# Attention in two-head matmuls, with v fetched once and copied on the chip

## The reference

```
for c in range(24):
    k_full = concat(mem_k, k[c*32-16 : c*32+40])      # 8 + 56 = 64 keys (fewer at both ends)
    v_full = concat(mem_v, v[same window])
    scores = q_c @ k_full.T / 8
    a = softmax(scores)
    out[chunk c] = a @ v_full
```

## Time and profile before

| | us |
|---|---|
| median of three runs | 758.82 |
| the profiled execution, whole | 762.52 |
| its span | 760.8 |
| attention, to the end of the last L616 | 241.5 |
| first mixture, to the last L761 | 329.2 |
| TensorE busy over the span | 642.0 (84%) |
| VectorE, ScalarE, GpSimd busy | 332.4, 228.0, 184.6 |

### The profile page before, as it was taken

How to read it: one execution, slowest core, us unless ns; L and a number is a source line. 1 busy time by engine, 2 the same in 40 slices (tenths; PEclk the granted TensorE clock), 3 DMA queues, 4 the chain that set the end, 5 groups by cost and what they waited for, 6 DMA issues and landing times.

```text
span 760.8 us, 18972 instructions
## 1 busy us (share of the span) xinstructions
PE 642.0 (84%) x6916; PEld 357.9 (47%) x6917; DVE 332.4 (44%) x543; ACT 228.0 (30%) x616; POOL 184.6 (24%) x159
## 2 busy tenths in 40 slices
PE   5999999699998969766430899999989999999992
PEld 3566666366665526433100445445444545444441
DVE  2333334133434652156370465665555566531120
ACT  2422424042422220010020344443434443443341
POOL 2211101010102000004786032332332233322221
PEclk9998999599999989897655799999999999999997
DMA  7769677558539999999805836455454543343332
GB/s 154 221 163 187 173 193 182 160 139 194 93 60 308 106 317 395 397 408 409 313 10 124 175 42 152 58 137 120 79 139 62 120 78 52 44 52 41 43 48 33
DMA packets 120601, 117.51 MB, mean 154 GB/s; under 512 B 57600, under 2 KB 87088, under 8 KB 120544
## 3 DMA queue, kind: packets, MB, share of 16 engines
q1 hardware_dynamic: 109104, 93.80, 42.1%
q0 software_dynamic: 11440, 22.87, 19.8%
HBM read 91.79 MB, written 22.76 MB: 151 GB/s over the span
## 4 chain that ended last, share of the span: by engine, by line
PE 57%; DMA 21%; issue 10%; DVE 3%; SPq 3%; ACT 3%; POOL 0%; ACTq 0%; DVEq 0%; POOLq 0%
PE ps L831 21%; DMA out_dram<-logits,arena 9%; DMA out_dram<-comb,arena 9%; PE ps L553 9%; PE ps L587 7%; PE ps L616 7%; DMA arena<-in_moe_w_dram 3%; PE ps L572 3%; PE ps L822 2%; PE ps L655 2%; PE ps L732 1%; SPq L418 1%; SPq L433 1%; ACT arena L920 1%; PE ps L761 1%
## 5 line engine op out<-in xcount | busy, mean ns | idle before, releaser
L831 PE MATMUL ps<-arena 128*128 x1320 | 300.2, 381 | 4.3 <-issue 3.5
L831 PEld LDWEIGHTS ps<-arena 128*128 128x128 f16 x1320 | 125.8, 98 | 143.6 <-issue 11.4
L1385 DVE SCALAR_TENSOR_TENSOR arena<-ps,arena 128x1024 f16<-128x1024 f32 x55 | 67.3, 1224 | 171.4 <-ACT arena L998 171.4
L998 ACT ACTIVATE arena<-ps 128x512 f16<-128x512 f32 x110 | 59.7, 594 | 130.3 <-PE ps L822 130.3
L553 PE MATMUL ps<-ident 128*128 128x128 f16 x384 | 90.9, 237 | 0.6 <-issue 0.5
L587 PE MATMUL ps<-arena 64*32 64x64 f32 x1536 | 72.1, 248 | 11.1 <-issue 11.1
L531 POOL DMA_INDIRECT out_dram<-logits,arena x28 | 47.9, 1710 | 123.6 <-DMA out_dram<-comb,arena 75.1
L531 POOL DMA_INDIRECT out_dram<-comb,arena x27 | 47.8, 1770 | 115.5 <-DMA out_dram<-logits,arena 90.7
L616 PE MATMUL ps<-arena 64*32 64x64 f32 x1536 | 65.5, 228 | 5.2 <-ACT arena L920 5.0
L468 POOL COPY arena<-arena 128x768 f32<-128x768 f32 x32 | 26.5, 828 | 173.8 <-PE ps L572 156.1
L522 POOL DMA_INDIRECT slot_table<-arena,zeros x48 | 51.5, 1072 | 29.8 <-DVE zeros L1283 15.5
(11 more groups left out here) (212 smaller groups left out, 577.9 us busy)
## 6 DMA issues: line engine op xcount, KB each, us to landing
arena<-in_moe_w_dram SPq DMA_DIRECT2D x26, 2048.0 KB, 18.7
arena<-in_moe_w_dram SPq DMA_DIRECT2D x12, 1024.0 KB, 5.8
arena<-in_v_dram SPq DMA_DIRECT2D x32, 308.0 KB
out_dram<-zeros POOLq DMA_DIRECT2D x2, 3200.0 KB, 18.7
arena<-in_q_dram SPq DMA_DIRECT2D x16, 384.0 KB, 4.5
arena<-in_k_dram SPq DMA_DIRECT2D x16, 384.0 KB, 5.0
arena<-arena SPq DMA_DIRECT2D x16, 128.0 KB
slot_table<-trow POOLq DMA_DIRECT2D x1, 935.0 KB, 38.1
```

Source lines behind the costliest of these rows:

```text
L831: last = mm(psY[par], hT[par][:, ph, c, :], W2[:, bass.ds(expert, 1), pw, c, :].rearrange("p o n -> p (o n)"), start=(c == 0 and ph == 0 a ...
L998: nc.scalar.activation(hT[par][:, 0, 4 * n:4 * n + 4, :].rearrange("p c n -> p (c n)"), psH[par][:, n, :], ACT.Relu).then_inc(relu_act, 1)
L1385: V.scalar_tensor_tensor(out=hT[i % 2][:, 1].rearrange("p c n -> p (c n)"), in0=psH[i % 2].rearrange("p a n -> p (a n)"), scalar=0.0, in1= ...
```

## The change

The two heads of a pair go into one matmul. `kB` holds the keys of head 0 in its rows 0 to 63 and of head 1 in rows 64 to 127, in two separate column ranges with zeros in the other half; `qT` has both heads in its 128 rows. A score matmul is now 128 rows by 32 columns with 2 x 56 columns moving. Six further matmuls with 128 columns of `qT` as the stationary operand give the scores of the 2 x 8 memory keys (`mkB`). `vB` is laid out in the same block-diagonal way, so that the product with v is 24 matmuls with 128 columns moving. The windows in `kB` need no copies of overlapping keys. The `keep_clock` matmuls are gone.

v is fetched in blocks of 64 tokens, each row once, 1536 packets per pair, which serves the even or odd chunks directly; the blocks of the other chunks are copied from it by VectorE (head 0) and ScalarE (head 1), new function `move_v`. The memory values are spread by GpSimd in two dependent copies (`spread_memv` moves there from VectorE). `qT`, `kB` and `aT` are single buffers. `load_v` now waits for the product of the pair two before; its first call waits until `vB` is zeroed.

```
-                sp.wait_ge(memv_spread, g + 1)
+                if not (isinstance(b, int) and b == 0 and m < 2):
+                    sp.wait_ge(pv_done, g - 1)
...
-                            (vW[i][lo + NM:lo + KEYS, 1:CH - 1, :],
-                             bass.AP(v_h.tensor, base + (CHUNK - LEFT) * D,
-                                     [[D, WIN], [CHUNK * D, CH - 2], [1, D]])),
+                            (vB[i][lo:lo + 64, EV + 1:VB - 1, own],
+                             bass.AP(v_h.tensor, base + (64 - NM - LEFT) * D,
+                                     [[D, 64], [64 * D, EV - 1], [1, D]])),
...
+            def spread_memv(b, m, after):                    # GpSimd
+                g, i = b * PPB + m, m % 2
...
+                pool.wait_ge(v_moved_dve, g + 1)
+                pool.wait_ge(v_moved_act, g + 1)
+                pool.wait_ge(memv_loaded[i], (b * (PPB // 2) + m // 2 + 1) * 32)
+                pool.wait_ge(k_ordered, after)
...
+                nc.gpsimd.tensor_copy(vB[i][0:NM, 0:CH, 0:D],
+                                      mvn[i][0:NM, :].unsqueeze(1).to_broadcast([NM, CH, D])
+                                      ).then_inc(memv_half, 1)
+                pool.wait_ge(memv_half, g + 1)
...
+                nc.gpsimd.tensor_copy(vB[i][64:64 + NM, 0:CH, D:2 * D],
+                                      mvn[i][64:64 + NM, :].unsqueeze(1).to_broadcast([NM, CH, D])
+                                      ).then_inc(memv_spread, 1)
...
             with pool.Fori(1, B) as b:
                 for m in range(PPB):
                     reorder(b, m)
+                    spread_memv(*((b, m - 2) if m >= 2 else (b - 1, m + PPB - 2)), b * PPB + m + 1)
+            spread_memv(B - 1, PPB - 2, PAIRS)
+            spread_memv(B - 1, PPB - 1, PAIRS)
             pool.wait_ge(scores_done, PAIRS)
...
-                    for h in range(2):
-                        lo = h * 64
-                        last = mm(psS[j * Q:(j + 1) * Q, h, t, :], qT[i][lo:lo + 64, c * CHUNK:(c + 1) * CHUNK],
-                                  kW[i][lo:lo + 64, c + 1, :], start=True, stop=True)
-                    if c % 2 == 0:
-                        keep_clock(2)
+                for t in range(ST):
+                    mm(psS[:, t // 3, t % 3, :, 0:NM], qT[:, t * P:(t + 1) * P],
+                       mkB[:, :, bass.ds(g * NM, NM)], start=True, stop=True)
...
+                    last = mm(psS[j * Q:(j + 1) * Q, t // 3, t % 3, :, NM:KEYS],
+                              qT[:, c * CHUNK:(c + 1) * CHUNK], kB[:, :, c * CHUNK:c * CHUNK + WIN],
+                              start=True, stop=True)
...
+                pe.wait_ge(memv_spread, g + 1)
...
+                    last = mm(psO[j * Q:(j + 1) * Q, t // 3, t % 3, :, :], aT[:, c * CHUNK:(c + 1) * CHUNK],
+                              vB[i][:, c // 2 + (1 - c % 2) * EV, :], start=True, stop=True)
...
+            def move_v(b, m):                                # ScalarE; VectorE does the same for head 0
+                i = m % 2
+                act.wait_ge(v_loaded[i], (b * (PPB // 2) + m // 2 + 1) * 96)
+                nc.scalar.copy(vB[i][64:96, 0:EV, D:2 * D], vB[i][96:128, EV:VB - 1, D:2 * D])
+                nc.scalar.copy(vB[i][96:128, 0:EV, D:2 * D], vB[i][64:96, EV + 1:VB, D:2 * D]
+                               ).then_inc(v_moved_act, 1)
...
+            V.memset(at(11, 0, 2 * PADDED), 0.0)
+            V.memset(mkB, 0.0).then_inc(kw_zeroed, 1)
+            V.memset(at(3, 0, 2 * VB * P), 0.0).then_inc(vb_zeroed, 1)
```

More of the change, by code:

```diff
@@ L342, in load_memv @@
                 i = m % 2
-                if isinstance(b, int) and b == 0 and m < 2:
-                    sp.wait_ge(mvn_zeroed, 2)
-                else:
+                if not (isinstance(b, int) and b == 0 and m < 2):
                     sp.wait_ge(memv_spread, g - 1)
@@ L464, in reorder @@
                     pool.wait_ge(done, (g + 1) * 16)
+                    if n == 0 and not first:
+                        if not (isinstance(b, int) and b == 0 and m < 3):
+                            pool.wait_ge(memv_spread, g - 2)
                     if not first:
@@ L613, in attend @@
                     t, j = c // CPT, c % CPT
-                    for h in range(2):
-                        lo = h * 64
-                        last = mm(psO[j * Q:(j + 1) * Q, h, t, :],
-                                  aT[lo:lo + 64, c * CHUNK:(c + 1) * CHUNK],
-                                  vW[i][lo:lo + 64, c, :], start=True, stop=True)
-                    if c % 2 == 0:
-                        keep_clock(6)
+                    last = mm(psO[j * Q:(j + 1) * Q, t // 3, t % 3, :, :], aT[:, c * CHUNK:(c + 1) * CHUNK],
+                              vB[i][:, c // 2 + (1 - c % 2) * EV, :], start=True, stop=True)
                 last.then_inc(pv_done, 1)
@@ L874, in _ @@
         def _(act):
+            act.wait_ge(kw_zeroed, 1)
             act.wait_ge(mkT_done, 1)
-            nc.scalar.copy(mkT[:, :], ps[:, 2, 0:P]).then_inc(mkT_ready, 1)
-            act.wait_ge(mkT_ready, 1)
+            for h in range(2):
+                own = slice(h * 64, h * 64 + 64)
+                nc.scalar.copy(mkB[own, h, :], ps[own, 2, 0:P]).then_inc(mkT_ready, 1)
             def copy_q(b, m):
                 g, i = b * PPB + m, m % 2
-                if not (isinstance(b, int) and b == 0 and m < 2):
-                    act.wait_ge(scores_done, g - 1)
+                if not (isinstance(b, int) and b == 0 and m < 1):
+                    act.wait_ge(scores_done, g)
                 for x in range(2):
@@ L931, in step @@
                     copy_k(*after)
-            act.wait_ge(kw_zeroed, 1)
+                if not (last and m == PPB - 1):
+                    move_v(*((b, m + 1) if m + 1 < PPB else (b + 1, 0)))
             copy_q(0, 0)
@@ L938, in _ @@
             exp(0, 0)
+            move_v(0, 0)
             for m in range(PPB):
@@ L1091, in step @@
                 norm(b, m)
-                if not (last and m >= PPB - 2):
-                    spread_memv(*((b, m + 2) if m + 2 < PPB else (b + 1, m + 2 - PPB)))
-            def spread_memv(b, m):
-                g, i = b * PPB + m, m % 2
-                dve.wait_ge(memv_loaded[i], (b * (PPB // 2) + m // 2 + 1) * 32)
-                V.tensor_copy(vW[i], mvn[i].unsqueeze(1).to_broadcast([P, CH, D])).then_inc(memv_spread, 1)
-            for i in range(2):
-                V.memset(mvn[i], 0.0).then_inc(mvn_zeroed, 1)
-            V.memset(at(11, 0, 2 * (CH + 2) * KEYS), 0.0).then_inc(kw_zeroed, 1)
-            dve.wait_ge(mvn_zeroed, 2)
-            spread_memv(0, 0)
-            spread_memv(0, 1)
+                if not (last and m == PPB - 1):
+                    move_v(*((b, m + 1) if m + 1 < PPB else (b + 1, 0)))
+            V.memset(at(11, 0, 2 * PADDED), 0.0)
+            V.memset(mkB, 0.0).then_inc(kw_zeroed, 1)
+            V.memset(at(3, 0, 2 * VB * P), 0.0).then_inc(vb_zeroed, 1)
+            move_v(0, 0)
             softmax(0, 0)
```

99 lines of the change are left out of this document (59 added, 40 removed).

## The result

The changed kernel takes **693.2 us** (median of 4 runs, 691.2 to 694.7) against 758.0 of the kernel before, measured with it: ratio 0.913, 95% interval 0.907 to 0.920. The forecast was 689, the range 666 to 722. The profiled execution took 692.8, with a span of 691.0. A few microseconds can only be compared within one series. Medians are over all executions of a kernel; the ratios leave out those that took over 1.5% more than its fastest.

A forecast was written before the change was run, and what follows sets the result against it. Attention was taken as bound by TensorE alone, DMA next. Old span 760.8, less 83.1 saved in attention, plus 11 given back, is 688.7, with 1.7 around it 690; median forecast 689 us, range 666 to 722.

The forecast's parts named there:

- TensorE in a new step: Attention step: product, scores, memory-key matmuls, transposes and two exposed hand-overs sum to 6.2 us, not setting the period.
- The chain of values: Attention, product to next product through normalization, v moves, GpSimd spreads and hand-overs: 7.3 us, the period of the last 4 steps.
- The period with weights: The 11 attention steps after the first product that carry weights take 8.2 us each, set by DMA.
- SyncE's queue: Issuing a pair's six v loads in attention takes SyncE 3.1 us, the same number of loads as before.
- DMA's own sum: DMA work per attention step for v, q and k, and weights: 7.75 us with weights, 5.3 without.
- Rival 1: In attention v comes late, making 11 steps 9.2 us each: 700 us, up to 715; chance 0.16.
- Rival 2: TensorE stays at 1.2 GHz in attention without `keep_clock`, 12.2 us a step: 754 us; chance 0.10.
- Rival 3: Attention matmuls' four column parts don't run side by side, 13.7 us a step: 779 us, slower; chance 0.04.
- Rival 4: Faster: attention has no stalls, DMA packs fully, 5 us are given back: 671 us; chance 0.10.
- The start: Zeroing, half-clock matmuls and the first v: first attention product done at 31 us, 10 before the old one.
- Stalls: 8 us added to attention for stalls of the same sort as before, which were 11 us then.
- Given back: After attention, zeroing starts later and pushes full DMA work behind attention, delaying the last expert's matrix: 11 us lost, bounds 0 and 11.5.

The follow-up runs named there:

- e12: Changed kernel without head 1's two copies of k on ScalarE (its scores made from zeros): 698.7 us in one run.
- e1: Changed kernel with the early expert-weight loads all moved into the last three steps: 718.0 us in one run.
- e2: Changed kernel without the two small v loads of each head from the third pair on (2 v DMAs a pair for 6): 698.1 us in one run.
- e14: Changed kernel plus unused filler matmuls on TensorE, 14 before the wait for copied k and 8 before that for spread memory values: 700.3 us, ratio 0.918.
- e18: The changed kernel, unchanged, run again in a later series: 704.0 us, ratio 0.924 to the kernel before.
- e6: Changed kernel with v's large DMAs moving 32 of the 64 columns, same packet count: 698.9 us in one run.
- e11: Changed kernel with ScalarE's copies of k placed ahead of the next pair's exponential: 715.8 us, ratio 0.932.
- e16: Changed kernel with the edits of e1, e11 and e14 joined: 717.5 us in one run.
- e17: Changed kernel with e14's filler, output zeroing issued once the last v landed, and every fourth step's early weights moved to the last three steps: 688.5 us, ratio 0.901.
- e3: Changed kernel with the v half undone: overlapping v windows fetched as before, no moves on the chip: 709.3 us, ratio 0.929.
- e4: Changed kernel with output zeroing issued before pair 14's memory-value spread and table clearing before the last spread: 721.7 us, ratio 0.946.

## Why the prediction was right, and where its sizes were off

- **TensorE in a new step**, forecast 6.2 us with 0.5 of hand-overs, so 5.7 of work: 6.85 in an undisturbed step. The product takes 1.52 (forecast 1.3), the scores 1.36 (1.15), the memory-key products 1.51 (1.3), the transposes 2.6 (2.0). Each group takes 0.2 more than I gave it, and this comes from the rows that I took it from. The earlier trace rows are pieces of the chain of waits, which counts 1.75 us for 32 matmuls and 0.66 for six transposes; the timeline of before has 1.96 and 0.87 for such groups:

```profile
327.21 1.96 PE L761 MATMUL ps<-arena,small 128*32 128x128 f32 x64 [0.23 <-DVE small L1200]
```

  It changes nothing in the forecast, in which TensorE does not set the period.
- **The chain of values**, 7.3: its parts were right (spread 2 x 1.46 = 2.9 for 3.3, moves 1.1 on VectorE for 1.0, ScalarE's 1.66), and the sum holds for the last steps of e12, 7.3 to 7.5 each. In the kernel after these took 8.1 on average, 7.3 and 7.5 the shortest.
- **The period with weights**, 8.2: the step that failed in size, 9.06. The term is "SyncE's queue: six v loads take 3.1, the same number as before". They take 5.2 to 6.9 in the nine weight steps from 52 us on, so SyncE's round is 9.1 in the step shown, where I had 3.1 for v and left the queue aside. e1 and e2 show that it would not have sufficed to ease this one: without it the scores' loop holds 8.5 at full clock, which I had not laid out at all. DMA's own sum was close: 0.91 x 9.06 = 8.2 us a step against 7.75, and 0.57 x 9.02 = 5.1 without weights against 5.3. That the DMA engines set the period, as forecast, is neither shown nor excluded: they have 0.91 of it, and their round and SyncE's were never told apart.
- **Rival 1**, v late at 9.2 a step, described the steps well: ScalarE and VectorE wait for v by name (20 and 9 us). Its period was nearer than the forecast's. Its road was not quite right, an issue of 3.1 and transfers queued ahead, and its time, 700, is 7 above the measured 693.2, because it too gave back 11 and added 8 of stalls.
- **Rival 2**: partly there and harmless. The granted clock is 0.93 over the steps with weights, and four products of 2.79 us (1.2 GHz) stand among twelve of 1.52 (2.4 GHz). The four follow waits of 2.23, 1.97, 0.77 and 4.30 us, but products at full clock follow waits of up to 2.14, so the wait just before does not tell which it will be. e14 raised the clock to 0.98, and the steps did not get shorter. The Trainium skill (TensorE: Matmul & The Clock Gate, A second HAM failure mode), which I had set beside it, describes a clock that goes to and fro between its two levels where TensorE idles shortly between groups, and the trace agrees in that.
- **Rival 3**: no, the product is 1.52, not 5.3. **Rival 4's** 671: no.
- **The start**, 31 us: 32.7. **Stalls**, 8: none is needed once the steps are 9.06 and 8.1; 32.7 + 11 x 9.06 + 4 x 8.1 and 1.3 for the last product's half clock make the 166.2. **The end of attention**, 158.4: 166.2.
- **Given back**, 11: 5.3. The zeroing starts 3 us before the end of attention, as forecast (2), and the waits for the layer's weights are 2.2 and 4.5 us, not one of 15. The full stretch from the zeroing to the last weight is 87.4 us (163.15 to 250.6) against 92.0 before (227.99 to 320.0), where I had taken it as fixed. The term is not firm: in e18 the stretch is 91.0 us (166.9 to 257.9) and 8.9 us are given back. The bandwidth over 92 us from the zeroing on, in 40 slices of 2.3 us, after:

```profile
GB/s 0 321 306 327 343 331 334 330 332 251 148 100 68 51 57 92 199 373 409 392 395 412 399 394 388 403 399 400 394 385 403 415 387 386 396 403 408 388 390 397
```

and before:

```profile
GB/s 143 328 329 331 331 335 294 347 334 244 127 92 42 55 41 43 30 21 217 408 394 390 385 420 415 386 389 393 407 402 389 387 402 411 392 388 394 410 396 392
```

  Both have a trough behind the zeroing, in which the engines are full and move little. The table's clearing (935 KB, 36.4 us from issue to landing) and the load of the noise (96 KB, 36.6 us) are under way there, and 1444 of the 1780 packets between 185 and 200 us are under 512 bytes. Slices below 110 GB/s were seven and are five, 4.6 us less, as much as the difference. Why it is shorter no run tells.
- So the sum came out within 0.6% by luck, because errors cancelled. The fifteen steps took 12.8 us more than forecast (11 x 0.86 and 4 x 0.84), and the start and the last product's half clock 3 more; the 8 us of stalls, which did not come, covered half of that. Attention saved 75.3 instead of 83.1, and 5.3 instead of 11 came back.

## What to carry over

When one engine's bound is lifted, lay out every loop that closes in one step, each through all its engines and the issue queue, before taking the next bound from busy shares. Here the chain of values has 7.4 us, the scores' loop 8.5 at full clock and the round of SyncE and the DMA engines 9.1. Six edits that each eased one limit (e1, e2, e6, e11, e12, e14) left it at 8.96 to 9.32 us, which is not to be told from the 9.06 to 9.36 of unchanged steps; e16 and e17, which eased several, have 8.79 and 8.69, 0.6 and 0.7 below the unchanged kernel on their chip. Take the length of an item from a timeline and not from a piece of the chain of waits, and that of DMA issues from rows where the queue is as full as it will be, and judge a change of an early stage by the point where the DMA-bound stage behind it ends.

## What the runs showed of the hardware that I had not expected

- The same loads take SyncE longer to issue when much is under way. Its six v issues took 3.1 to 4.1 us before (the earlier trace rows has 3.14, at a DMA share of 0.75 from 172 to 178 us). The same windows in e3, at 0.98 between 41 and 151 us, took 7.2 to 10.6. The new, smaller loads took 3.9 and 4.2 at first, 5.2 to 6.9 from 52 us on while weights came (5.74 at 90.89, share 0.98 in that step), 3.27 in the last two steps (0.31 at 141.7), and 12.14 behind the zeroing of 6.4 MB in e4. The share alone does not fix it: the issue at 134.41 of the kernel after took 3.73 at 0.96.
- In e4 v was asked for from 2 us after that zeroing on, and it landed so late that its reader waited 28.3 us.
- A copy over 8 partitions on GpSimd is no cheaper than its row length says: 8x1536 in 1.46 us, 128x768 in 0.82.
- The same unchanged kernel had medians of 693 and 704 us in two series, and the same steps took 9.06 to 9.36 us in four executions.
